# Reordering copies, tanh and layer pieces in the dense slots of a fused attention and two-layer kernel

## Reference

```python
scores = scale * np.matmul(q, k.transpose(0, 1, 3, 2))
...
attn = np.exp(scores)
attn = attn / (np.sum(attn, axis=-1, keepdims=True) + 1e-09)
return np.matmul(attn, v).astype(np.float32)
...
h = x @ w_in
g = h - np.tanh(h)
return (g @ w_out).astype(np.float32)
```

## Time and profile before

| | us |
|---|---|
| three runs | 1223.7, 1225.61, 1226.31 |
| median | 1225.61 |
| the profiled execution | 1224.13 |
| its span, first to last instruction | 1222.2 |
| mean granted TensorE clock | 0.997 |
| busy: PE, DVE, ACT, POOL | 1178.2, 595.8, 569.6, 531.5 |

### The profile page before, as it was taken

The page is one execution under the profiler, slowest core; times in us unless marked ns, Lnnn a source line. Parts: engine busy times, 40 slices in busy tenths (PEclk is TensorE's granted clock), DMA queues, the critical chain, the costliest instruction groups (busy, mean ns, idle before and its releaser), DMA issues.

```text
span 1222.2 us, 20183 instructions
## 1 busy us (share of the span) xinstructions
PE 1178.2 (96%) x7320; PEld 1080.2 (88%) x7320; DVE 595.8 (49%) x1377; ACT 569.6 (47%) x1163; POOL 531.5 (43%) x584
## 2 busy tenths in 40 slices
PE   6769899999999999999999999999999999999998
PEld 2346699999999998999899999999999999999998
DVE  8957777756565657666666534321211212122111
ACT  7968577655565556556555554422211222121212
POOL 0048677765666657777878522111111111111111
PEclk9989999999999999999999999999999999999999
DMA  6878464444343434455555344100000000000000
GB/s 198 277 238 260 141 190 139 126 128 119 111 143 113 116 97 141 132 145 135 154 135 140 123 135 149 52 26 27 27 1 27 26 26 26 1 26 1 26 1 26
DMA packets 77763, 125.46 MB, mean 103 GB/s; under 512 B 17120, under 2 KB 40672, under 8 KB 77664
## 3 DMA queue, kind: packets, MB, share of 16 engines
q1 hardware_dynamic: 77664, 124.16, 34.2%
HBM read 104.07 MB, written 20.05 MB: 102 GB/s over the span
## 4 chain that ended last, share of the span: by engine, by line
PE 83%; DVE 10%; issue 3%; ACT 2%; POOL 1%; DMA 1%; SPq 0%; DVEq 0%; POOLq 0%; ACTq 0%
PE ps_y L1484 14%; PE ps_h L1465 13%; PE ps_s L1586 12%; PE ps_y L1597 12%; PE ps_h L1586 6%; PE ps_pt L1586 6%; PE ps_s L1382 6%; PE ps_pt L1436 5%; PE ps_pt L1401 5%; DVE feat L1090 4%; PE ps_pt L1465 1%; DVE prob L1125 1%; DVE fr L1175 1%; DVE wbuf L1141 1%; ACT prob L804 1%
## 5 line engine op out<-in xcount | busy, mean ns | idle before, releaser
L739 POOL TENSOR_TENSOR fr<-tanh_b,fr 128x384 fp32r<-128x384 f32 x72 | 73.2, 1017 | 377.9 <-ACT fr L1017 377.9
L1484 PE MATMUL ps_y<-fr,wbuf 128*128 128x384 f32 x1152 | 230.4, 337 | 0.0
L1465 PE MATMUL ps_h<-fr,wbuf 128*128 128x384 f32 x1056 | 206.1, 338 | 1.5 <-DVE fr L1175 1.1
L1484 PEld LDWEIGHTS ps_y<-fr,wbuf 128*128 128x128 f32 x1152 | 198.2, 188 | 0.8 <-POOL fr L681 0.8
L1465 PEld LDWEIGHTS ps_h<-fr,wbuf 128*128 128x128 f32 x1056 | 181.6, 188 | 3.3 <-issue 1.8
L804 ACT ACTIVATE prob<-prob,negmax 128x576 f32<-128x576 f32 (+1 forms) x160 | 124.0, 775 | 115.2 <-DVE negmax L1125 114.7
L676 POOL TENSOR_SCALAR prob<-prob,rowinv 128x576 f32<-128x576 f32 (+1 forms) x160 | 127.6, 799 | 110.2 <-DVE rowinv L1136 110.2
L1597 PE MATMUL ps_y<-wbuf,fr 128*128 128x512 f32 x648 | 161.1, 393 | 0.0
L681 POOL TENSOR_TENSOR fr<-g_b,fr 128x384 fp32r<-128x384 f32 x96 | 100.6, 1048 | 115.8 <-ACT fr L835 115.8
L1597 PEld LDWEIGHTS ps_y<-wbuf,fr 128*128 128x128 f32 x648 | 120.5, 188 | 22.1
L1125 DVE CUSTOM_DVE_ANT_0 prob<-ps_s,biasb 128x576 f32<-128x576 f32 (+1 forms) x147 | 110.0, 748 | 13.7 <-PE ps_s L1382 12.5
(11 more groups left out here) (134 smaller groups left out, 1946.0 us busy)
## 6 DMA issues: line engine op xcount, KB each, us to landing
biasb<-bias_scratch SPq DMA_DIRECT2D x64, 288.0 KB, 3.2
raw<-k_t SPq DMA_DIRECT2D x59, 288.0 KB, 3.1
biasb<-bias_scratch SPq DMA_DIRECT2D x64, 216.0 KB, 2.8
bias_scratch<-w_raw SPq DMA_DIRECT2D x72, 144.0 KB, 3.2
biasb<-bias_scratch SPq DMA_DIRECT2D x64, 144.0 KB, 2.9
w_raw<-w_chunks SPq DMA_DIRECT2D x16, 512.0 KB, 5.2
prob<-w_chunks SPq DMA_DIRECT2D x8, 768.0 KB, 4.8
raw<-v_p SPq DMA_DIRECT2D x36, 160.0 KB, 2.3
```

Source lines behind the costliest of these rows:

```text
L1465: mm = eng.matmul(hidden_bank(u, c)[:, 0:TOK], w[:, cols], x[:, d, :], start=d == 0 and i == 0, stop=d == KC - 1 and i == 2)
L1484: mm = eng.matmul(ps_y[:, d, 0:TOK], w[:, cols], g[c % 2], start=c == 0 and i == 0, stop=c == C1 - 1 and i == 2)
```

## The change

On ACT, exp of head 8's third tile moves from the first dense slot to the end of `edge`. In the first dense slot the first copy of the transposes goes ahead of tanh, on DVE `inverse(v, 2)` and `pt_low` ahead of `gated`, on POOL `split_v` ahead of `split_g`, and PE makes the second and third tiles' transposes directly behind the scores of the tile before, with two pieces ahead of the scores that follow. In the ordinary slots the second copy goes ahead of tanh and g_high behind the third copy, and on DVE the second `pt_low` and `score` go ahead of `gated`. In the first slots of units 1 and 2 PE makes three old pieces, not two, before the new unit's, and the end's copy goes ahead of q_high. In the first short slots the gaps are 5 and 1 pieces, not 4 and 2, and the last `y_out` and `o_part` go ahead of exp of the second tile.

```diff
@@ -697,9 +697,9 @@
                     for u, c in moe:
                         split_g(u, c)
                     return
+                split_v(v)
                 if v.n == H:
                     split_g(*moe[0])
-                split_v(v)
                 if len(moe) == 1:
                     if begins(moe):
                         split_k(p, moe)
@@ -890,6 +890,7 @@
                 exp_tile(q, 1)
                 o_part(v, moe)
                 q_high(p, moe)
+                exp_tile(q, 2)
 
             def dense_alone(moe):
                 u, s = moe[0][0], moe[0][1] // 2
@@ -910,12 +911,11 @@
                     pt_high(v, 1, moe)
                     exp_tile(q, 0)
                     q_high(p, moe)
-                    y_out(u - 1, [1, 2])
+                    y_out(u - 1, [1, 2, 3])
+                    o_part(v, moe)
                     exp_tile(q, 1)
-                    o_part(v, moe)
                     tanh(u, c)
                     g_high(u, c)
-                    y_out(u - 1, [3])
                     return
                 if p is not None:
                     q_high(p, moe)
@@ -941,35 +941,38 @@
                     short(q, v, p, moe)
                     return
                 u, tiles, first = moe[0][0], w1_tiles(moe), begins(moe)
+                pt_high(v, 0, moe)
                 if v.n == H:
                     tanh(*moe[0])
-                pt_high(v, 0, moe)
-                if v.n == H:
                     g_high(*moe[0])
-                    exp_tile(v, 2)
-                if first:
+                    pt_high(v, 1, moe)
+                    exp_tile(q, 0)
+                elif first:
                     y_out(u - 1, [0])
-                exp_tile(q, 0)
-                if not first and v.n > H:
-                    tanh(*moe[0])
-                pt_high(v, 1, moe)
-                if first:
+                    exp_tile(q, 0)
+                    pt_high(v, 1, moe)
                     tanh(*moe[0])
                     y_out(u - 1, [1])
                     pt_high(v, 2, moe)
-                if v.n > H:
                     g_high(*moe[0])
-                if first:
                     y_out(u - 1, [2])
+                else:
+                    exp_tile(q, 0)
+                    pt_high(v, 1, moe)
+                    tanh(*moe[0])
                 exp_tile(q, 1)
                 if first:
                     y_out(u - 1, [3])
+                    pt_high_end(v)
                 else:
                     pt_high(v, 2, moe)
+                    if v.n > H:
+                        g_high(*moe[0])
                 q_high(p, moe)
                 for k in tiles[-1:]:
                     w1_high(k)
-                pt_high_end(v)
+                if not first:
+                    pt_high_end(v)
                 for k in tiles[0:2]:
                     w1_high(k)
                 for t in range(2, q.nt):
@@ -1271,19 +1274,28 @@
                     return
                 u, tiles, first = moe[0][0], w1_tiles(moe), begins(moe)
                 if v.n == H:
+                    inverse(v, 2)
+                    pt_low(v, 0, moe)
                     gated(*moe[0])
-                pt_low(v, 0, moe)
-                if v.n == H:
-                    inverse(v, 2)
-                score(q, 0, moe)
-                inverse(q, 0)
-                if not first and v.n > H:
-                    gated(*moe[0])
-                pt_low(v, 1, moe)
-                score(q, 1, moe)
-                if first:
+                    score(q, 0, moe)
+                    pt_low(v, 1, moe)
+                    inverse(q, 0)
+                    score(q, 1, moe)
+                    inverse(q, 1)
+                elif first:
+                    pt_low(v, 0, moe)
+                    score(q, 0, moe)
+                    inverse(q, 0)
+                    pt_low(v, 1, moe)
+                    score(q, 1, moe)
                     gated(*moe[0])
                 else:
+                    pt_low(v, 0, moe)
+                    score(q, 0, moe)
+                    inverse(q, 0)
+                    pt_low(v, 1, moe)
+                    score(q, 1, moe)
+                    gated(*moe[0])
                     inverse(q, 1)
                 pt_low(v, 2, moe)
                 if not first:
@@ -1532,7 +1544,7 @@
                 if begins(moe) and len(moe) == 2:
                     (u, c), (_, c1) = moe
                     left, new = model_pieces(u - 1, C1 - 1), hidden_pieces(u, c)
-                    pieces = left[:2] + new[:2] + new[2:] + left[2:] + hidden_pieces(u, c1) + model_pieces(u, c)
+                    pieces = left[:3] + new + left[3:] + hidden_pieces(u, c1) + model_pieces(u, c)
                 for u, c in [] if pieces else moe:
                     if c > 0:
                         pieces += hidden_pieces(u, c) + model_pieces(u, c - 1)
@@ -1543,16 +1555,30 @@
                     for _ in range(min(k, len(pieces))):
                         pieces.pop(0)()
 
-                gaps = [4, 2] if len(moe) == 1 else [4, 4, 2] if begins(moe) else [4, 3, 3]
-                after_end = 3
                 if moe[0] == (0, 0):
                     layer_work(3)
-                    gaps, after_end = [2, 2, 1], 1
+                    transposed(v, 0, moe)
+                    layer_work(1)
+                    scores(q, 0, moe)
+                    transposed(v, 1, moe)
+                    layer_work(2)
+                    scores(q, 1, moe)
+                    transposed(v, 2, moe)
+                    layer_work(2)
+                    scores(q, 2, moe)
+                    transposed_end(v, moe)
+                    layer_work(2)
+                    output(v, moe)
+                    layer_work(len(pieces))
+                    return
+                gaps, after_end = [4, 3, 3], 3
+                if begins(moe):
+                    gaps = [5, 1] if len(moe) == 1 else [4, 4, 2]
+                elif len(moe) == 1:
+                    gaps = [4, 2]
                 for t, gap in enumerate(gaps):
                     if t < v.nt:
                         transposed(v, t, moe)
-                    if moe[0] == (0, 0) and t == 0:
-                        layer_work(1)
                     if q is not None and t < q.nt:
                         scores(q, t, moe)
                     layer_work(gap)
```

## The result

The changed kernel takes 1221.57 us (median of 12 runs, 1220.75 to 1222.78), the kernel before beside it 1224.55 (median of 12): ratio 0.9975, 95% interval 0.9966 to 0.9984, or **2.98 us faster**. The profiled execution took 1221.89 us with a span of 1220.0, where before's had 1224.13 and 1222.2.

What follows compares the result with a forecast made beforehand. TensorE, busy 96% of the span, was taken as the bound, leaving only its idle time and stalls to win. Gains 1.7 + 1.5 + 0 + 1.3 + 0.86 + 0.14 = 5.5 us, from 1225.61 to 1220.1, range 1216.5 to 1223.5.

Steps and rivals of the forecast that it cites:

- A: First dense slot: end transposes and output come earlier; gain 1.7 us, floor 1.0, ceiling 2.6.
- C: First slots of units 1 and 2: shorter waits of the new unit's piece and the output; 0.65 us each, 1.3 together.
- D: First short slots of units 3 and 4: y_out out of the copy's way, gated earlier; 0.43 us each, 0.86 together.
- B: Seven ordinary slots of unit 0: third scores 0.37 us sooner each; net gain 1.5 us, bounds 0 to 2.6.
- The replay's chain: First dense slot, replayed: copies, exps and reductions lead to end transposes at 139.0 and output at 140.75.
- The gross: Unit 0's ordinary slots: third scores 0.37 us sooner in seven slots, 2.5 us before 1.0 is taken back.
- The price of the end's copy and q_low: Unit 0's ordinary slots: g_high delays the end's copy 0.10 us, split_g delays q_low 0.05; 7 x 0.15 = 1.0 lost.
- taken back: First short slots: the fifth piece's 0.2 us at the output is lost when the next slot's hidden pieces wait for gated.
- Only the first slot pays: Rival, chance 0.13: third-transposes gains return as stalls at slot ends, first slots stay bound by DVE reductions; 1.7 + 0.4, 1223.5 us.
- Slower: Rival, chance 0.04: split_g holds q_low 0.51 us longer in all 21 ordinary slots, 10.7 us against 5.5 won; 1230.8 us.

Runs made afterwards that it cites:

- after_short_w1: Changed kernel with GpSimd's w1 subtraction replaced by a shorter one-input write of 0 x the high part: 1218.53 us (one run), unit 0's seven slots 94.31.
- ordinary_as_before: Changed kernel with the ordinary slots' old order on ScalarE and VectorE put back: 1221.27 us (9 runs), ratio to the kernel before 0.9973.
- ordinary_alone: Kernel before with only the ordinary slots' new order on ScalarE and VectorE: 1224.77 us (11 runs), ratio 1.0004.
- norm_before_g: Changed kernel with GpSimd's norm of the second tile ahead of split_g in the ordinary slots: 1224.15 us (11 runs), ratio 0.9997.
- w1_later: Changed kernel with two w1 subtractions of each unit 0 slot, one GpSimd's and one VectorE's, made in the next slot: 1220.32 us (5 runs), ratio 0.9967.

## Why the prediction was right and where it was wrong

Forecast 1220.1 within 1216.5 to 1223.5, faster with 0.81: it came out at 1221.57, faster. Of the 5.5 us gain 3.0 came: the mechanism held for A, C and D, and B gave nothing.

- **First dense slot**: 1.7 forecast, 1.87 found. The replay's chain holds: end transposes 139.43 - 0.49 = 138.94 against 139.0, output 140.66 against 140.75. Moving exp into the slot before cost nothing.
- **Ordinary slots of unit 0**: 1.5 forecast, -0.25 found. The gross was right: 2.63 at the third scores and 2.37 by the slots' ends between the kernels with the short subtraction, against 2.5. **The step that failed** is "norm, split_k and the w1 subtraction, queued behind split_g on POOL, come up to 1.2 later and are wanted in the next slot only, 1.3 or more after", and so priced at nothing. The lateness was even more: against the next slot's first transposes L687 came 1.8 later in one slot looked at (184.93 for 185.94, where it had been 184.59 for 187.41). But I asked only who needs their results. Nobody did; what they cost is DVE's time, since POOL's w1 subtraction now starts ahead of DVE's pair and holds it, ahead of the first pt_low, where before it started behind DVE's first one and was itself held. after_short_w1 puts 2.67 us on it, and ordinary_as_before shows that the net is zero.
- **The price of the end's copy and q_low**, 7 x 0.15: q_low was indeed held by split_g (1.07, not 0.56), but with both in place after_short_w1 had as much gained at the output as at the third scores, 2.63, so they cost nothing there; 0.26 in all went behind the output, where 1.0 was forecast. That error hid part of the other: the loss that I had not seen was 2.67.
- **Units 1 and 2, ordinary**: 0 forecast, 0.04 and 0.19 found. 0.12 of the latter are unit 2's last slot (0.14 forecast), 0.10 in ordinary_alone, so it is the new order's.
- **Their first slots**: 0.65 each forecast, 0.56 and 0.60 found; PE's part 0.18 and 0.20 (forecast 0.17), the copy's 0.39 and 0.43 (forecast 0.53 less 0.05).
- **Short slots**: 0.43 each forecast, 0.45 and 0.44 found, but by other shares, and that the sum fits is partly luck: y_out out of the way was to give 0.37 and PE's order next to nothing ("taken back"); everything but PE's order gave 0.28, PE's order alone 0.16. Then the second step that failed: "No DMA issue moves by more than its releaser; SP's queue keeps its order." Both halves are true, and still the load of k came late: y's store moved up with its releaser by 1.3 us against the slot, into the bias loads. I had not asked what stands behind it in the queue. That took 1.1 back in unit 4. Unit 3's third slot lost nothing: its load took 4.7 instead of 3.7 and still landed 0.3 sooner against the slot.
- **The rivals.** "Only the first slot pays" is wrong on C and D. It is right that B gave nothing, but not by its mechanism, the end's copy behind g_high. The mechanism of "Slower" was one POOL instruction away: norm_before_g shows it, at about 0.14 a slot in unit 1 instead of 0.51, because only the part past the end's copy counts.

The point missed by 1.5 us. The range held because A, C and D came as forecast: B's -0.25 lies below its own floor of 0, and the 1.1 of unit 4's third slot was in no bound.

## What to carry to other kernels

When a move makes an engine's queue later, list not only who waits for its results but which instructions of other engines now run beside it: here a DVE instruction with two inputs in SBUF (the on-chip working memory) and a POOL one that read SBUF took nearly the time of one after the other, and which of them paid changed with every shift of either queue. Test a reorder together with the place of the background work (here the w1 subtractions): moving it gave 3.5 us in the old order (96.73 to 93.24) and 0.7 in the new one (96.98 to 96.32). A store that is released sooner can delay a load behind it in its queue, as in unit 4: put the load with a deadline first.

## What the runs showed of the hardware

**DVE and POOL exclude each other, both ways.** In the changed kernel DVE's w1 subtraction started first and POOL's split_k was held, 1.93 us instead of 1.43:

```profile
183.00 0.69 DVE L1085 TENSOR_TENSOR wbuf<-w_raw,wbuf 128x512 fp32r<-128x512 f32 x1
...
183.04 1.93 POOL L660 TENSOR_TENSOR fr<-raw,wbuf 128x576 fp32r<-128x576 f32 x1
```

In w1_later split_k started first (181.62) and the subtraction was held, 1.85 instead of 0.69 (above): 1.16 more, where 1.43 - 0.12 = 1.31 of split_k were left. What is added is what is left of the first one, less about 0.15, in all six pairs shown: 0.50 of 0.65 (split_k above), 0.46 of 0.60 (L687 at 184.59 in the kernel before), 1.16 of 1.31, 0.82 of 0.96 and 0.50 of 0.64 (q_low behind split_g at 291.81 and 290.63), and 0.32 of 0.45 (L658 at 292.74 behind q_low, 0.99 instead of 0.67). The last has a single tensor input, so on POOL one is enough. The Trainium skill, "SBUF — State Buffer", section "Who interferes with whom", calls the shared port pair an exclusive lock, says that a DVE instruction with two SBUF inputs contends for it with a GpSimd one that reads SBUF, and that issue order, not the operation's shape, decides who is blocked; by that rule the trace agrees. I had used it for q_low alone. By it every two-input DVE instruction in the slot was to be set against POOL's new places, which is the step that failed.

**A load behind a store on one queue** landed after 6.2 us instead of 4.2, while the store itself, issued straight behind the bias loads, took 6.0 instead of 4.0; ahead of the store the load took 4.5 and the store 5.5. The Trainium skill, "DMA: Bandwidth & Descriptors", section "Queues, rings and completion order", says that a transfer's completion is written only after every earlier write of the same DMA engine; that fits a load that can't be seen to land ahead of the store, but no run here tells it from plain sharing of the DMA engines, and it stays open. So does why that landing, and with it the third slot of unit 4, spreads by 0.9 us between kernels that don't differ there, and whether the new order with w1 work at yet another place would beat the 93.24 us of the old one; that was not tried.
